# Gate group 0 split by GpSimd in the last head, and head 0's scores placed inside the last folding tile's products

## The reference

```python
# attention, B=2, 16 heads in all, S=768, head dim 64
mask   = q_bucket[:, :, :, None] == k_bucket[:, :, None, :]   # 6 sign bits of q@proj, k@proj
scores = where(mask, q @ k^T / sqrt(D), -1e9)
attn   = exp(scores - max) / (sum + 1e-9)
x      = (attn @ v) as [1536, 512]
# gated layer, d_ff = 1024
a = x @ w1 ; b = x @ w2
y = ((a * b) @ w3) @ w_out
# 4 weighted experts
out = sum_e p[:, e] * (relu(y @ W1[e]) @ W2[e])
```

## Time and profile before

| | |
|---|---|
| median of the runs | 1011.39 us |
| the profiled execution | 1012.22 us |
| its span in the profile | 1010.4 us |
| TensorE clock granted | full in all 40 slices |
| PE / weight loads / DVE / ACT / POOL busy | 98% / 91% / 63% / 46% / 40% |
| DMA | 60 GB/s mean |

### The profile page before, as it was taken

One profiled execution on the slowest core, in us unless ns is written; L12 is line 12 of the kernel. 1 busy time (PEld: TensorE's weight loads), 2 busy tenths in 40 slices (PEclk: granted clock), 3 DMA queues, 4 the chain that ended last, 5 costly groups with the idle time before them and its releaser, 6 DMA issues.

```text
span 1010.4 us, 15884 instructions
## 1 busy us (share of the span) xinstructions
PE 991.1 (98%) x5504; PEld 922.2 (91%) x5504; DVE 638.6 (63%) x965; ACT 462.9 (46%) x855; POOL 405.8 (40%) x412
## 2 busy tenths in 40 slices
PE   7999999999999999999999999999999999999998
PEld 5879999999988999999998998989989899898997
DVE  5338999999997998298855354453534536345342
ACT  3328888888886554354543140431504215042230
POOL 4022243385544994394445060341603416043130
PEclk9999999999999999999999999999999999999999
DMA  6322333433332221011020110201102011010102
GB/s 240 95 70 79 111 100 90 117 99 94 86 104 80 63 63 43 22 43 29 14 64 21 42 43 1 63 21 43 43 1 62 21 42 42 6 57 21 42 13 111
DMA packets 58925, 60.58 MB, mean 60 GB/s; under 512 B 7808, under 2 KB 46848, under 8 KB 58880
## 3 DMA queue, kind: packets, MB, share of 16 engines
q1 hardware_dynamic: 58880, 60.00, 20.0%
HBM read 44.20 MB, written 3.19 MB: 47 GB/s over the span
## 4 chain that ended last, share of the span: by engine, by line
PE 90%; DVE 6%; issue 2%; ACT 1%; DMA 1%; SPq 0%; DVEq 0%; ACTq 0%
PE ps L287 23%; PE ps L288 22%; PE ps L289 22%; PE ps L1376 6%; PE ps L1363 3%; PE ps L1365 3%; PE ps L1389 3%; PE ps L1391 3%; PE ps L1341 2%; PE ps L1336 2%; DVE w_lo L1014 2%; DVE hid_lo L1138 1%; DVE pT_lo L998 1%; DMA w_raw<-in_moe_w 1%; PE ps L1300 1%
## 5 line engine op out<-in xcount | busy, mean ns | idle before, releaser
L602 POOL TENSOR_TENSOR v_sum<-kept,kept 128x384 f32<-128x384 f32 x48 | 52.6, 1095 | 292.3 <-ACT kept L793 292.3
L1270 DVE SCALAR_TENSOR_TENSOR acc<-ps,gate,acc 128x512 f32<-128x512 f32 x96 | 72.0, 750 | 135.8 <-PE ps L289 135.8
L793 ACT COPY kept<-ps 128x384 f32<-128x384 f32 x144 | 64.2, 480 | 199.1 <-PE ps L289 198.5
L289 PE MATMUL ps<-v_hi,hid_lo 128*128 128x512 f32 x384 | 149.6, 390 | 0.0
L288 PE MATMUL ps<-v_lo,hid_hi 128*128 128x512 f32 x384 | 149.5, 389 | 0.0
L287 PE MATMUL ps<-v_hi,hid_hi 128*128 128x512 f32 x384 | 149.4, 389 | 0.0
L980 DVE TENSOR_SCALAR_CACHE_REDUCE expo<-ps 128x768 f32<-128x768 f32 x96 | 91.6, 954 | 18.9 <-PE ps L1365 18.5
L690 ACT ACTIVATE expo<-expo,neg_max 128x768 f32<-128x768 f32 x96 | 90.6, 944 | 9.7 <-DVE expo L980 8.2
L1257 DVE SCALAR_TENSOR_TENSOR hid_lo<-c,hid_hi 128x384 fp32r<-128x384 f32 x96 | 63.1, 669 | 46.2 <-ACT hid_hi L914 19.1
L698 ACT CAST pT_hi<-ps 128x768 fp32r<-128x768 f32 x96 | 76.9, 802 | 31.4 <-PE ps L1376 30.9
L998 DVE TENSOR_TENSOR pT_lo<-ps,pT_hi 128x768 fp32r<-128x768 f32 x96 | 90.4, 946 | 1.4 <-ACT pT_hi L698 1.3
(11 more groups left out here) (155 smaller groups left out, 2509.1 us busy)
## 6 DMA issues: line engine op xcount, KB each, us to landing
w_raw<-in_moe_w SPq DMA_DIRECT2D x64, 128.0 KB, 2.4
e_raw<-in_moe_w SPq DMA_DIRECT2D x64, 128.0 KB, 2.3
v_raw<-in_moe_w SPq DMA_DIRECT2D x32, 256.0 KB, 3.2
w_raw<-in_moe_w SPq DMA_DIRECT2D x8, 512.0 KB, 4.0
raw_q<-in_q SPq DMA_DIRECT2D x16, 192.0 KB, 2.9
raw_k<-in_k SPq DMA_DIRECT2D x16, 192.0 KB, 2.8
raw_v<-in_v SPq DMA_DIRECT2D x16, 192.0 KB, 2.7
q_main<-q_cross SPq DMA_DIRECT2D x16, 192.0 KB, 2.7
```

Source lines behind the costliest of these rows:

```text
L289: return nc.tensor.matmul(out_ps, lhs_lo, rhs_hi, start=False, stop=stop, skip_group_check=onto)
L602: nc.gpsimd.tensor_tensor(v_sum[:, :], kept[s][1][:, :], kept[s][2][:, :], ALU.add).then_inc(v_done, 1)
L793: nc.scalar.copy(kept[s][n][:, :], ps[4 * s + n][:, 0:HALF]).then_inc(kept_done, 1)
L1270: nc.vector.scalar_tensor_tensor(acc[:, t, :], ps[4 * ((h + t // 4) % 2) + t % 4], gate_f[:, bass.ds(t * E + e, 1)], acc[:, t, :], ALU.mul ...
```

## The change

Three edits.

1. Group 0's high and low parts are made by POOL, right after it has made the sums of groups 0 and 1: cast of 1024 columns, subtraction of 1024, cast of 768, subtraction of 768. ACT's two casts and DVE's two subtractions of that group are gone. Two new semaphores (`first_hi_done`, `first_lo_done`) take their place, and the counts of `w_lo_done` and `w_hi_done` waited for by the others are lower by one group.
2. Of head 0, scores 0 to 3 are issued inside the last folding tile, ahead of `kt` = 1, 3, 5 and 7. Before, scores 0 and 1 stood ahead of `kt` = 2 and 5, scores 2 behind the tile and scores 3 at the head of the attention code.
3. The last preparation step of head 1 (second half of its one-hot code) moves from the head of the last folding tile to just ahead of `kt` = 2, and DVE's scaling of scores 0 moves ahead of that step's DVE part.

```diff
@@ SP
             def load_gate(g):
-                if g >= RAWS:
-                    sp.wait_ge(w_lo_done, 2 * (g - RAWS) + 2)
+                if g == RAWS:
+                    sp.wait_ge(first_lo_done, 2)
+                elif g > RAWS:
+                    sp.wait_ge(w_lo_done, 2 * (g - RAWS))
@@ POOL, behind combine_gate(0), combine_gate(1)
+            pool.wait_ge(prep_mm, GROUPS * (HEADS - 1) + 4)
+            pool.wait_ge(k_split, HEADS)
+            pool.wait_ge(score_mm, TILES * (HEADS - 1))
+            for n, (lo, hi) in enumerate(((0, 4), (4, 7))):
+                pool.wait_ge(w_combined, 3 + n)
+                nc.gpsimd.tensor_copy(w_hi[0][:, lo:hi, :], w_raw[0][:, lo + 1:hi + 1, :]).then_inc(first_hi_done, 1)
+                pool.wait_ge(first_hi_done, n + 1)
+                nc.gpsimd.tensor_tensor(w_lo[0][:, lo:hi, :], w_raw[0][:, lo + 1:hi + 1, :],
+                                        w_hi[0][:, lo:hi, :].bitcast(F32), ALU.subtract).then_inc(first_lo_done, 1)
@@ ACT, attention
-                    def first_weights(part):
...
-                            gate_high(0, *((0, 4, 3), (4, 7, 4))[part])
...
                     pT_high(6 * m + 3, 3)
-                    first_weights(0)
...
                     exp(1, 0)
-                    first_weights(1)
                     pT_high(6 * m + 5, 5)
@@ DVE, attention and behind it
                     pT_low(6 * m + 4, 4)
-                    if last and s == 1:
-                        gate_low(0, (1,))
...
             attention(PAIRS - 1, False, True)
-            gate_low(0, (2,))
             o_sum(2 * HEADS - 2, PAIRS - 1, 1, 0, ps_o)
@@ DVE, folding
                 wp_low(it - 1, (it - 1) % 2)
+                if it == FK - 1:
+                    scale_scores(0, 0)
                 first_code(2 * it - 1)
...
-            scale_scores(0, 0)
             scale_scores(1, 1)
@@ PE, multiply_wp
-                    if it == FK - 1 and kt in (2, 5):
-
-                        scores(kt // 3, 0, 0, kt // 3, kt == 2)
+                    if it == FK - 1 and kt % 2:
+
+                        scores(kt // 2, 0, 0, kt // 2, kt == 1)
+                    if it == FK - 1 and kt == 2:
+                        first_prep(2 * it - 1)
@@ PE, attention and folding
-                    score(0, 3)
+                    if not (first and s == 0):
+                        score(0, 3)
...
-                first_prep(2 * it - 1)
+                if it < FK - 1:
+                    first_prep(2 * it - 1)
...
-            scores(2, 0, 0, 2, False)
```

More of the change, by code:

```diff
@@ L253, in build_program @@
         w_combined, w_hi_done, w_lo_done = sem("w_combined"), sem("w_hi_done"), sem("w_lo_done")
+        first_hi_done, first_lo_done = sem("first_hi_done"), sem("first_lo_done")
         e_combined, e_hi_done, e_lo_done = sem("e_combined"), sem("e_hi_done"), sem("e_lo_done")
@@ L358, in load_expert @@
                         sp.wait_ge(prod, N_PROD * GATE_ALL)
-                        sp.wait_ge(w_lo_done, 2 * GATE_ALL)
+                        sp.wait_ge(w_lo_done, 2 * (GATE_ALL - 1))
                         sp.wait_ge(ab_done, 3 * GATE_UNITS)
@@ L1007, in o_sum, with gate_low @@
                                         bank[0:DH, 0:HALF], o_low[:, :], ALU.add).then_inc(o_full_done, 1)
-            def gate_low(g, parts=(1, 2)):
+            def gate_low(g):
                 if g < GATE_ALL:
-                    for part in parts:
-                        lo, hi = (0, 4) if part == 1 else (4, 7)
-                        dve.wait_ge(w_hi_done, 2 * g + part)
+                    for part, lo, hi in ((1, 0, 4), (2, 4, 7)):
+                        dve.wait_ge(w_hi_done, 2 * (g - 1) + part)
                         nc.vector.tensor_tensor(w_lo[g % SLOTS][:, lo:hi, :], w_raw[g % RAWS][:, lo + 1:hi + 1, :],
@@ L1502, in gates @@
                         parts = {k: (xg_lo_done, k + 1) for k in range(N_PROD)} if b else {0: (xf_done, 18)}
-                    products(step, s % 2, 0, (w_hi[step % SLOTS], w_lo[step % SLOTS]), w_lo_done, step, parts)
+                    products(step, s % 2, 0, (w_hi[step % SLOTS], w_lo[step % SLOTS]),
+                             w_lo_done if step else first_lo_done, max(step - 1, 0), parts)
             def multiply_y(b):
```

## The result

| | before | after |
|---|---|---|
| median of 22 runs each | 1011.33 us (1010.58 to 1012.85) | 1009.99 us (1008.53 to 1011.73) |
| ratio, 95% interval | | 0.9986 (0.9979 to 0.9992) |
| profiled execution / its span | 1012.22 / 1010.4 us | 1008.62 / 1006.8 us |

The change takes about 1.3 us off, 0.14%: clear of the interval, but within the 0.2% that the prediction called no change. The forecast was 1009.9. The two spans differ by 3.6 us, much more than the medians, so the first thing to find is what of it the change made. I cut every profile at four instructions of PE: S, the first one-hot step ahead of the last folding tile; P, the first gate product; Y, the first product with `wp_hi`; X, the first expert product. The change touches nothing ahead of S. In the table "seam" is the second and third edit together, "GpSimd part" the first; the columns are in us.

A forecast was written before the change was run, and what follows sets the result against it. PE, working 98% of the 1010.4 us span, was taken as the bound, so only its idle time could be won. Seam 1.1 + last head 0.2 + gate groups 0.2 = 1.5 us, from 1011.39 to 1009.9 us; range 1008.8 to 1011.3.

The forecast's parts named there:

- The seam, 1.1 us: From folding to attention: scores 4 start at 73.77 instead of 74.90, a shift of 1.1 us kept afterwards.
- The margin of 0.16 us for the scaling: Last folding tile: score tiles start 2.08 us apart against 1.92 needed for scaling, so PE does not wait.
- The end of the last head, 0.2 us: Last head: POOL's last subtraction holds up DVE's guard, leaving 0.2 us gain; bounds +0.8 and -0.65.
- The gate groups, 0.2 us: Gate groups: POOL's earlier start takes back between nothing and 0.98 us of PE's waits; 0.2 us taken.
- a new pattern of collisions: Gate groups, DVE and POOL running nearly without a gap: new collisions could add 0.3 us.
- The sum: Whole kernel: 1.1 + 0.2 + 0.2 = 1.5 us gained, span 1008.9, median 1009.9 us.
- The guard not held up: Rival, last head: guard undelayed, gain there 0.8, total 2.1 us, time 1009.3; chance 0.13.
- The seam giving half: Rival, seam: PE stalls at two score tiles, leaving 0.5 there, total 0.7 us, time 1010.7; chance 0.17.
- The gate groups giving back their waits: Rival, gate groups: 1.0 us gained there, total 2.3 us, time 1009.1; chance 0.12.
- Slower: Rival, seam: scores 1, 2 and 3 each wait 1.2 us for scaling, time 1013.5; chance 0.05 including other slowdowns.

The follow-up runs named there:

- experiment 1: Kernel before with only the seam edits (scores 0 to 3, one-hot step and scaling moved): 1010.47 us, ratio 0.9990 to before.
- experiment 8: Changed kernel with its third edit undone, so the second one-hot step stays ahead of the last folding tile: 1009.81 us, one run.
- e12: Changed kernel, nothing edited, measured a third time: 1009.57 us, ratio 0.9981 to before.
- e11: Changed kernel with GpSimd's second cast (768 columns) made twice, so its last subtraction ends later: 1012.01 us, one run.
- experiment 2: Changed kernel with the seam edits undone, leaving only group 0's parts on GpSimd: 1011.97 us, ratio 1.0009 to before.
- experiment 3: Changed kernel with DVE's guard in the last head moved behind the low part of tile 3: 1010.32 us, ratio 0.9990 to before.
- experiment 4: Changed kernel, nothing edited, measured again: 1011.09 us, ratio 0.9996 to before.
- experiment 6: Changed kernel with VectorE's product made to wait for GpSimd's in the second pair of gate steps: 1011.65 us, ratio 1.0003 to before.
- experiment 7: Seam edits alone, plus head 0's scores 4 ahead of tile 1's transposes and scaling 3 ahead of the last wp_lo: 1008.87 us, ratio 0.9976 to before.
- experiment 5: Changed kernel with GpSimd's product made to wait for VectorE's in the second pair of gate steps: 1009.14 us, ratio 0.9977 to before.
- experiment 9: Changed kernel with scores 4 earlier, the last head's guard later, and VectorE's product forced ahead of GpSimd's: 1007.70 us, ratio 0.9958 to before.
- experiment 10: Changed kernel without the seam edits, with VectorE's product forced ahead of GpSimd's in the second gate pair: 1010.13 us, ratio 0.9986 to before.

## Why the prediction was right, step by step

- **The seam, 1.1 us: right.** 1.16 in after, 1.15 in experiment 1. Scores 4 stand 11.11 us behind S, where the sum had 73.77 - 62.63 = 11.14. The margin of 0.16 us for the scaling held. Of the two causes the sum did not say which carried it; experiment 8 says that the one-hot step's move does, with 1.0.
- **The end of the last head, 0.2 us: mechanism right, size off.** From the start of the transposes ahead of this place to the end of PE's last wait there it took 6.60 us before (311.55 to 318.15) and takes 6.01 after (308.76 to 314.77): 0.6 us. The guard was held as said. The term that was mis-sized is the end of POOL's last subtraction: I took a start at 307.70 and 1.11 + 2.47 for the 1024-column pair; the pair started about 307.5 on the clock of before (304.73 + 311.55 - 308.76) and took 1.04 and 2.41. So the last subtraction ended 0.35 us sooner, the guard lasted 0.69 and not 1.0, and it delayed `pT_lo` by 0.25 and not 0.65.
- **The gate groups, 0.2 us: right in the middle, wrong in its shape.** I gave -0.3 to +0.98 and chose a value near nothing, from a chain of waits, as if the outcome were one number. It is at least three, as a gain from P to Y: +0.47 with VectorE ahead (after), -0.35 with GpSimd ahead once (e12), -1.4 with GpSimd ahead twice (e11, whose extra cast is in the last head). The earlier start of POOL's row, foreseen as harmless or good, brings its product from P + 33.1 to P + 31.6, on top of DVE's. POOL's sums begin 1.15 us earlier against P (4.24 us behind it before, 3.09 in after), where I had 0.5 to 1. I had named "a new pattern of collisions" as the lower bound and not looked for its place, though the order and the durations were in the trace.
- **Behind X** I had nothing. In after PE waits 0.36 us for `kept` 89.4 us behind X, and before has no wait there. Experiments 2, 3, 4, 6, 8 and 12 have it; 1 and 7, without the GpSimd part, don't, nor do 5, 9, 10 and 11, which add an instruction to GpSimd's program. The rows lead back to one idle time of POOL, first before, then after, with PE's wait:

```profile
590.91 1.01 POOL L608 TENSOR_TENSOR c<-u_sum,v_sum 128x384 f32<-128x384 f32 x1 [0.27 <-POOL v_sum L602]
...
587.36 1.01 POOL L621 TENSOR_TENSOR c<-u_sum,v_sum 128x384 f32<-128x384 f32 x1 [0.56 <-POOL v_sum L615]
...
592.93 0.42 PE L288 MATMUL ps<-early_hi,e_hi 128*128 128x384 f32 x1 [0.36 <-ACT kept L796]
```

At this place POOL is idle for 0.56 us in the seven profiles that have PE's wait, and for 0.27 in the seven that don't; ACT's `hid_hi` behind it, and `kept` after that, are late by the same 0.3. Why POOL starts later there is open. Part of what experiments 5 and 10 gain comes from there.
- **The sum.** By the profiles, 1.16 + 0.59 + 0.47 - 0.3 = 1.9 us where VectorE wins the tie, and 1.16 + 0.59 - 0.35 - 0.3 = 1.1 where GpSimd wins it once. The medians' difference is 1.34, the forecast was 1.5. That it came out so close is partly luck, because two misses were opposite: 0.4 too little in the last head, and 0.3 lost behind X with part of the runs on the losing side of the tie.
- **The rivals.** The guard not held up: fallen (0.69, 1.40). The seam giving half: fallen. The gate groups giving back their waits: half true, in the executions where VectorE wins (0.22 and 0.76 have become 0.27). Slower: not so for the whole, but experiment 2 shows that the GpSimd part alone is not faster while the tie is open.

That the order of the two products moves the time is shown by force (experiments 5, 6 and 10), and by the rows of seven profiles. That it makes the whole spread of the open kernel is not shown: with VectorE forced ahead the spread is 1.8 us in each of two sets of 11, much as that of before (1.5 to 2.5 in its sets of 15 to 33), but with GpSimd forced ahead it is 3.5, and S alone moves by 1.75. What decides an open tie is not shown either: the two products start within 0.01 us, in either order.

## What to carry to other kernels

Work moved to GpSimd can be paid for where VectorE's SBUF-only instructions meet it, even the tiny ones, so go through the order behind the change and look for two long SBUF-only instructions that become ready together; then give the one whose successor PE waits for the precedence, by a semaphore. Where a median and a profile disagree, or a kernel's runs spread more than their neighbours', profile the same kernel again before explaining: one profile is one outcome. Cut spans at instructions ahead of and behind the change before comparing them; 1.6 of the 3.6 us here had nothing to do with it.

## What the runs showed of the hardware

- Two SBUF-only products of 128x384, started within 0.01 us of one another on VectorE and GpSimd, don't share: 0.56 and 1.44 us when VectorE is ahead, 1.42 and 1.01 when GpSimd is. Both outcomes come from the same program (after and experiment 12).
- A VectorE instruction of 128x6 is held for the rest of a GpSimd subtraction: 0.69 and 1.40 us (after, experiment 11) in place of 0.15 to 0.16. Each held one ends 0.02 to 0.04 us behind the subtraction. In before, too, seven of the 16 guards are held and last 0.66 to 1.82 us; what these cost was not tried. `pT_lo`, which has one input in PSUM and one in SBUF, takes 0.90 to 0.96 in all 96 cases of every profile, beside GpSimd or not.
- GpSimd's time does not grow quite as the width: a cast takes 0.84 us at 768 columns and 1.04 at 1024, a subtraction 1.82 and 2.41 (after).
- The stretch ahead of the last folding tile ends at 61.05 to 62.80 us in 14 executions that run the same code up to there.
